# Linear attention ahead of an MLP: queries laid out by feature block and transposed on VectorE, key sums and token sums in column halves of the array

## The reference

```python
# 1: linear attention, per batch and head
q_s = exp(q - max(q, over the 64 features));  q_s /= sum(q_s, over the features) + 1e-9
k_s = exp(k - max(k, over the 576 tokens));   k_s /= sum(k_s, over the tokens) + 1e-9
kv  = k_s^T v                    # 64 x 64 per head
x   = q_s kv                     # 576 x 64 per head; the heads side by side give 576 x 512
# 2: x = x + relu(layernorm(x) * g @ w_ch1) @ w_ch2           (512 -> 2048 -> 512)
# 3: four experts, each a 64-wide causal attention over x; the best two of four by a gate are added
```

## Time and profile before

| | |
|---|---|
| median of three runs | 1400.9 us |
| the profiled execution | 1399.72 us, its span 1397.9 us |
| mean granted TensorE clock | 0.984 |
| PE busy | 1328.8 us, 95% |
| VectorE (DVE) busy | 663.0 us, 47% |
| ScalarE (ACT) busy | 498.0 us, 36% |
| GpSimd (POOL) busy | 229.6 us, 16% |
| DMA | 70.48 MB, 147018 packets, 126704 of them under 512 B |

### The profile page before, as it was taken

The page is one execution under the profiler, slowest core; times in us unless marked ns, Lnnn a source line. Parts: engine busy times, 40 slices in busy tenths (PEclk is TensorE's granted clock), DMA queues, the critical chain, the costliest instruction groups (busy, mean ns, idle before and its releaser), DMA issues.

```text
span 1397.9 us, 19591 instructions
## 1 busy us (share of the span) xinstructions
PE 1328.8 (95%) x7392; PEld 1153.6 (83%) x7392; DVE 663.0 (47%) x1628; ACT 498.0 (36%) x1092; POOL 229.6 (16%) x260
## 2 busy tenths in 40 slices
PE   4699999999999999999999999998799999999996
PEld 3577888888888888888888888887789999999984
DVE  5776344244234244244244122113677767767662
ACT  3343122122122122122122111112456666666663
POOL 0221000000000000000000000012555535543231
PEclk9899999999999999999999999999899999999998
DMA  8441410410500500600600100302112012101101
GB/s 158 125 103 67 94 35 0 105 33 8 113 17 0 128 10 8 128 1 0 136 1 8 61 0 9 97 1 77 41 35 69 24 46 69 42 28 35 34 31 38
DMA packets 147018, 70.48 MB, mean 50 GB/s; under 512 B 126704, under 2 KB 130800, under 8 KB 146928
## 3 DMA queue, kind: packets, MB, share of 16 engines
q1 hardware_dynamic: 140672, 67.66, 19.5%
q10 hardware_dynamic: 6256, 1.57, 0.7%
HBM read 49.29 MB, written 19.92 MB: 50 GB/s over the span
## 4 chain that ended last, share of the span: by engine, by line
PE 89%; DVE 4%; issue 3%; ACT 1%; POOL 1%; SPq 1%; DMA 1%; POOLq 0%; DVEq 0%; ACTq 0%
PE hb L1207 28%; PE yb L1306 27%; PE sc L1207 19%; PE ob L1444 3%; PE tb L1426 3%; PE pa L1207 2%; PE pa L1242 2%; PE yb L1294 1%; PE pa L1270 1%; PE pa L1256 1%; DVE w_lo L889 1%; DMA qsb<-in_q_dram 1%; POOL prob L635 1%; PE yb L1336 0%; SPq L415 0%
## 5 line engine op out<-in xcount | busy, mean ns | idle before, releaser
L1008 DVE SCALAR_TENSOR_TENSOR hid_lo<-hb,hid_hi 128x512 fp32r<-128x512 f32 x144 | 99.5, 691 | 454.8 <-ACT hid_hi L712 454.5
L712 ACT ACTIVATE hid_hi<-hb 128x512 fp32r<-128x512 f32 x144 | 86.0, 597 | 541.0 <-PE hb L1207 541.0
L1306 PE MATMUL yb<-hid_hi,w_hi 128*128 128x512 f32 x576 | 232.6, 404 | 0.0
L1207 PE MATMUL hb<-xn_hi,w_hi 128*128 128x512 f32 x576 | 228.2, 396 | 1.4 <-issue 1.4
L1306 PE MATMUL yb<-hid_hi,w_lo 128*128 128x512 f32 x576 | 225.0, 391 | 0.0
L1207 PE MATMUL hb<-xn_hi,w_lo 128*128 128x512 f32 x576 | 224.7, 390 | 0.0
L1306 PE MATMUL yb<-hid_lo,w_hi 128*128 128x512 f32 x576 | 224.5, 390 | 0.0
L1207 PE MATMUL hb<-xn_lo,w_hi 128*128 128x512 f32 x576 | 224.4, 390 | 0.0
L1306 PEld LDWEIGHTS yb<-hid_hi,w_lo 128*128 128x128 f32 x576 | 108.1, 188 | 23.4
L1207 PEld LDWEIGHTS hb<-xn_hi,w_lo 128*128 128x128 f32 x576 | 108.2, 188 | 23.2
L1207 PEld LDWEIGHTS hb<-xn_hi,w_hi 128*128 128x128 f32 x576 | 108.3, 188 | 23.0 <-issue 1.7
(11 more groups left out here) (180 smaller groups left out, 2366.1 us busy)
## 6 DMA issues: line engine op xcount, KB each, us to landing
y_scratch<-ysb SPq DMA_DIRECT2D x36, 256.0 KB, 2.8
qsb<-in_q_dram SPq DMA_DIRECT2D x32, 256.0 KB, 4.9
stage<-in_moe_w_ch_dram SPq DMA_DIRECT2D x16, 512.0 KB, 4.4
out_dram<-osb SPq DMA_DIRECT2D x32, 256.0 KB, 2.0
y_in<-y_scratch SPq DMA_DIRECT2D x28, 288.0 KB, 3.9
ksb<-in_k_dram SPq DMA_DIRECT2D x31, 256.0 KB, 4.5
vsb<-in_v_dram SPq DMA_DIRECT2D x28, 256.0 KB, 4.5
vsb<-in_v_dram ACTq DMA_DIRECT2D x4, 256.0 KB, 7.4
```

Of the source, the lines that this page charges most:

```text
L712: act.activation(HID[f % 2][0][:], hb[f % 2][:], ACT.Relu).then_inc(sems["hhi_a"], 1)
L1008: dve.scalar_tensor_tensor(out=lo[:], in0=hb[f % 2][:], scalar=0.0, in1=plain(hi[:]), op0=ALU.max, op1=ALU.subtract).then_inc(sems["hlo_v" ...
L1207: ins = pe.matmul(dst, l, r, start=(n == 0), stop=(n == len(terms) - 1))
L1306: ins = pe.matmul(yb[j][:], l, r, start=False, stop=(f == FT - 1 and m == 2), skip_group_check=True)
```

## The change

* **Queries.** They are loaded as `qx[128, 4, 18, 32]`: partition = (half of the heads, half of the features, token mod 32), then head in its half, block of 32 tokens, feature in its half. A DMA moves runs of 32 floats (128 B) in place of 64 (256 B), 4 DMAs of 32 partitions per batch, and each batch carries its own 576 tokens. The maximum over a row is one `tensor_reduce` over 32 features, an exchange of partition blocks (4 copies of 72 columns) and a `max`. VectorE transposes 32 x 32 blocks in place (`qT`), after which features are on partitions. TensorE's query transposes, ScalarE's copies to `qeT` and the step `qsum` are gone.
* **Key sums.** Head x * 4 + g goes to column half x of the array: 40 matmuls of 64 weight columns and 65 moving ones in place of 20 of 128 and 130. The last tile uses 64 rows.
* **Token sums.** Weights are 64 query tokens of one pair of heads (g and g + 4), the moving side `KV[:, g]` with 130 columns: kv of both heads and a column of ones for each, which yields the query sums. Per token tile 4 x 2 matmuls in alternating column halves; for the tail tile 4, all in the upper half.
* **Tokens.** A tile's step `tokens` on VectorE is an add, a reciprocal and two multiplications, and then the statistics as before. The tail goes to rows 64 to 127 of `ksb` and is stored per batch. There is no X5; `qT` stands at half 15 and `kvn` at 16 (it was 15); `ln`, `xn` and T0 to T3 stand one half earlier.
* **Buffers.** x has a buffer of its own (`xsb`), kmx lies in it; `kvbd` is one buffer `KV`; a pad keeps the place of the weights.

```diff
-        q_v = q.rearrange("(p x) h s d -> x p s h d", x=2)
+        q_v = q.rearrange("(p x) (y g) (n r) (z c) -> x p y z r g n c", x=2, y=2, r=32, z=2)
...
-        ORDER = ["kmx0", "kmx1", "kmaxT", "kbc", "ksub0", "ksub1", "qmax", "qsub0", "qsub1", "kv", "kvn", "qsum",
-                 "X0", "X1", "X2", "X3", "X4", "X5", "ln", "xn", "T0", "T1", "T2", "T3"]
+        ORDER = ["kmx0", "kmx1", "kmaxT", "kbc", "ksub0", "ksub1", "qmax", "qsub0", "qsub1", "kv", "qT", "kvn",
+                 "X0", "X1", "X2", "X3", "X4", "ln", "xn", "T0", "T1", "T2", "T3"]
...
+                for b in range(4):
+                    sp_.dma_start(qx[b * 32 : (b + 1) * 32], q_v[st[1], st[0], b // 2, b % 2]).then_inc(q_in, 16)
...
+            def store_tail(st):
+                need(sp_, "x_v", st, NT)
+                sp_.dma_start(xt_dram[st[0], st[1] * TAIL : (st[1] + 1) * TAIL], ksb[P - TAIL : P, CT, :]).then_inc(xt_out, 16)
...
+            def tokens(st, t, sums):
+                r = slice(P - ROWS[t], P)
+                need(dve, "x_mm", st, t + 1)
+                heads = sums[r, :, 0 : 4 * (HD + 1)].rearrange("p b (n c) -> p b n c", c=HD + 1)
...
+                dve.tensor_scalar(xrs[r].rearrange("p b (n o) -> p b n o", o=1), heads[:, :, :, HD : HD + 1], EPS_SUM, None, ALU.add).then_inc(sems["xrs_v"], 1)
+                need(dve, "xrs_v", st, 2 * t + 1)
+                dve.reciprocal(xrs[r], xrs[r]).then_inc(sems["xrs_v"], 1)
+                need(dve, "xrs_v", st, 2 * t + 2)
...
+                for x in range(2):
+                    ins = dve.tensor_tensor(to.rearrange("p (x b n d) -> p x b n d", x=2, b=2, n=2)[:, x], heads[:, :, x::2, 0:HD],
+                                            xrs[r, :, x::2].rearrange("p b (n o) -> p b n o", o=1).to_broadcast([ROWS[t], 2, 2, HD]), ALU.mult)
+                ins.then_inc(sems["x_v"], 1)
...
                 if s == "qmax":
+                    dve.wait_ge(q_in, st[0] * (8 * 16) + (st[1] * 64 + 64))
+                    for n in range(2):
+                        dve.tensor_reduce(qmx[:, 2 * n * NG : (2 * n + 2) * NG], qx[:, 2 * n : 2 * n + 2].rearrange("p g n c -> p (g n) c"), AX.X, ALU.max).then_inc(sems["qmx_v"], 1)
...
+                    for b in range(4):
+                        dve.tensor_copy(other[32 * b : 32 * b + 32], qmx[32 * (b ^ 1) : 32 * (b ^ 1) + 32]).then_inc(sems["qmx_v"], 1)
+                    need(dve, "qmx_v", st, 6)
+                    dve.tensor_tensor(qmx[:], qmx[:], other, ALU.max).then_inc(sems["qmx_v"], 1)
...
+                if s == "qT":
+                    for g in range(HP):
+                        need(dve, "qexp_a", st, g + 1)
+                        dve.transpose(q_part(g), q_part(g)).then_inc(sems["qT_v"], 1)
...
+            def key_sums(dst, vs, t):
+                for g in range(HP):
+                    for x in range(2):
+                        h = x * HP + g
+                        ins = pe.matmul(dst[x * HD : (x + 1) * HD, g * (HD + 1) : (g + 1) * (HD + 1)],
+                                        ksb[0 : ROWS[t], t, h * HD : (h + 1) * HD], vs[0 : ROWS[t], t, h, :],
+                                        start=(t == 0 and g == 0), stop=(t == NT - 1), skip_group_check=True)
+                return ins
...
+            def token_sums(dst, t):
+                for g in range(HP):
+                    for n in (0, 1) if t < CT else (1,):
+                        at = 4 * t + 2 * n if t < CT else 4 * t
+                        ins = pe.matmul(dst[n * HD : (n + 1) * HD, X_BANK[g], g % 2 * 2 * (HD + 1) : (g % 2 + 1) * 2 * (HD + 1)],
+                                        qx[:, g, at : at + 2, :], KV[:, g], start=True, stop=True)
+                return ins
...
                 if s[0] == "X":
...
                     t = int(s[1])
+                    need(pe, "qT_v", st, HP)
+                    if t == 0:
+                        need(pe, "kv_v", st, 2)
+                    else:
+                        need(pe, "x_v", st, t)
+                    token_sums(PA, t).then_inc(sems["x_mm"], 1)
...
             low_piece(0)
             inverse_deviation(START)
             step("xn", START)
+            tokens(START, CT, FIRST_X[CT])
```

More of the change, by code:

```diff
@@ L84, in program @@
         ksb = sb("ksb", [P, NT, D], F32, st1)
[L85 to L88, removed]
+        NG = S // 32
+        qx = sb("qx", [P, HP, NG, 32], F32, st1)
+        with ExitStack() as st:
+            kmx = sb("kmx", [P, D], F32, st)
+        xsb = sb("xsb", [P, CT, D], F32, st1)
+        KV = sb("kv", [P, HP, 2, HD + 1], F32, st1)
+        sb("pad", [P, 248], F32, st1)
         v_and_xn(0)
@@ L386, in items @@
                 return [s for s in LAST_ORDER if LAST_HALF[s] == h]
-            return [s for s in ORDER if HALF[s] == h and (s != "X5" or st[1])]
+            return [s for s in ORDER if HALF[s] == h]
         def is_last(st):
@@ L897, in token_stats, with normalize_kv @@
                 dve.bn_aggr(mv[:, t, :], bst[:, t, :]).then_inc(sems["mv_v"], 1)
-            def normalize_kv(st, first, rest):
+            def normalize_kv(st, sums):
                 need(dve, "kv_mm", st, 1)
[L901 to L904, removed]
+                kv = sums[:, 0:KVW].rearrange("p (g c) -> p g c", g=HP)
+                dve.tensor_scalar(krs[:].rearrange("p (g o) -> p g o", o=1), kv[:, :, HD : HD + 1], EPS_SUM, None, ALU.add).then_inc(sems["krs_v"], 1)
+                need(dve, "krs_v", st, 1)
+                dve.reciprocal(krs[:], krs[:]).then_inc(sems["krs_v"], 1)
@@ L905, in normalize_kv @@
                 need(dve, "krs_v", st, 2)
[L906 to L912, removed]
+                for x in range(2):
+                    h = slice(x * HD, (x + 1) * HD)
+                    dve.tensor_tensor(KV[h, :, x, 0:HD], kv[h, :, 0:HD], krs[h].rearrange("p (g o) -> p g o", o=1).to_broadcast([HD, HP, HD]), ALU.mult).then_inc(sems["kv_v"], 1)
@@ L967, in step @@
                 if s == "kvn":
-                    normalize_kv(st, pa[0][:, 0 : 3 * KVW], pa[1][:, 0:KVW])
-                if s == "qsum":
-                    need(dve, "qexp_a", st, queries(st))
-                    for t0, t1 in groups(st):
-                        dve.tensor_reduce(stat(qrs, t0, t1), per_head(qsb, t0, t1), AX.X, ALU.add).then_inc(sems["qrs_v"], 1)
-                    need(dve, "qrs_v", st, 2 + st[1])
-                    every = stat(qrs, 0, queries(st))
-                    dve.tensor_scalar(every, every, EPS_SUM, None, ALU.add).then_inc(sems["qrs_v"], 1)
-                    need(dve, "qrs_v", st, 3 + st[1])
-                    dve.reciprocal(every, every).then_inc(sems["qrs_v"], 1)
@@ L1036, in _ @@
                 step(s, START)
-            normalize_kv(START, FIRST_KV[0][:, 0 : 3 * KVW], FIRST_KV[1][:, 0:KVW])
-            step("qsum", START)
+            normalize_kv(START, FIRST_KV)
+            step("qT", START)
             for t in range(CT):
-                need(dve, "x_mm", START, t + 1)
-                need(dve, "qrs_v", START, 4)
-                dve.tensor_tensor(per_head(qsb, t, t + 1), FIRST_X[t][:].rearrange("p (h d) -> p h d", d=HD), spread(qrs, t, t + 1), ALU.mult).then_inc(sems["x_v"], 1)
-                need(dve, "x_v", START, t + 1)
-                token_stats(START, t)
+                tokens(START, t, FIRST_X[t])
             variance(START)
```

206 lines of the change are left out of this document (74 added, 132 removed).

## The result

Twenty runs of the changed kernel have a median of 1403.45 us (1400.31 to 1408.03). Nineteen of the kernel before have 1399.89 (1398.87 to 1401.77; one more run, of 2696 us, is left out). That is +3.6 us against a forecast of +0.6: inside the range of 1394 to 1412, on the slower side of the 0.2% that I called no change. The profiled execution took 1405.98 us with a span of 1403.9, so it stands 2.5 us above its median. The one before had 1399.7 and 1397.9.

A forecast was written before the change was run, and what follows sets the result against it. The prediction took the array (PE) as the bound, except where VectorE's chain leads in START and the first chunk. 1399.7 + 6.0 + 2.3 - 7.7 = 1400.3, with 1.2 for the median 1401.5 us; range 1394 to 1412.

The forecast's parts named there:

- no change: Whole kernel: a difference within about 0.2%, 2.8 us, can't be told from none; the forecast itself, chance 0.34.
- The six later chunks: Chunks after the first that carry an attention: PE time saved by cheaper key sums and token products, net -7.7 us.
- The stall of 1 us ahead of X0: Later chunks: the first token product comes 0.1 to 0.2 us late, waiting for kvn; 6 x 0.17 = 1 us.
- The start interval of 55 ns: Array passes start at most every 55 ns or so, key sums keep 4.45 us; time 1410.2 us, chance 0.20.
- The faster rival: Short passes of the key sums run at full rate, 2.3 us; time 1397.3 us, chance 0.28.
- START: Stretch before the first chunk: q's landing and VectorE's chain grow, +6.0 us (ends +3 and +10).
- The price of q: START: 14.4 ns per 128 B packet makes q's load 8.3 us instead of 4.9, +3.4 us.
- my lower end: START: q's load priced by bytes alone, +0.6 us.
- The first chunk: VectorE nearly full, token products and T0 come later, PE's saving turns into waiting; +2.3 us (ends +0.5 and +5).
- VectorE in front at double price: START and first chunk: block transposes cost twice the price, +2.4 us each; 1406.3 us, chance 0.18 shared with dear q.

The follow-up runs named there:

- warm: Changed kernel with 15 extra fp32 products of a zero matrix ahead of X0, X2 and T0 of the first chunk; 1399.46 us, 0.9989 of before.
- first_later: Changed kernel with kvn and all steps that follow it one to three halves later in the first chunk alone; 1391.56 us, 0.9942 of before.
- keysums: Kernel before with the key sums alone in column halves, keys, queries and tokens as they were; 1385.11 us, 0.9898 of before.
- best_a: keysums_all with 30 extra matmuls ahead of START's transposes; 1385.24 us, 0.9887 of before.
- ksub_first: Changed kernel with the key subtraction ahead of the query maximum in START; 1400.81 us, 1.0007 of before.
- q_256: Changed kernel with q loaded in runs of 256 B, leaving out the right placement of q; 1402.13 us, 1.0022 of before.
- keysums_all: keysums with the key subtraction first in START and a later order in the first chunk; 1381.36 us, 0.9872 of before.

## Why the prediction came out as it did

**The six later chunks, -7.7 for -8.6: right, by its mechanism.** Key sums 3.0 (measured 2.86 with the switch), token tiles 1.23 (1.30), a batch 9.5 (9.4 by the same rows). The stall of 1 us ahead of X0 did not come; without it the sum is -8.7. The start interval of 55 ns was my slower rival; passes 31 and 33 ns apart, 80 in a row, rule it out. The Trainium skill (TensorE: Matmul & The Clock Gate, Wait — 56ns, not 53.3ns?) gives some 62 ns per MATMUL where hardware decoding is off; at 31 ns per pass that bound doesn't act here. The faster rival's 2.3 for the key sums was too low, though nearer than mine on the passes alone (2.63).

**START, +6.0 for a measured +5.8: right sum by luck, wrong terms.** The profiled executions part as follows. q landed 0.8 later (predicted 3.4). qmax until ksub took 1.4 more (1.1). From there to the first token tile it was 0.5 less (1.2 less). The missing 0.7 is mostly the key sums: they ended 6.3 us after ksub began, where I had 5.65, and VectorE waited 0.6 for them. It isn't the clock of the token product, 2.01 us at a granted clock of 0.50, which was in my sum. The key sums themselves took 4.82 us at a granted clock of 1.00, while ScalarE, which feeds them, was busy for 4.96 of the 5 us from 25 to 30. The four token tiles took 2.4 more (2.0), and the fifth, behind xn, 0.1 (0.7). The first 24 MLP matmuls took 7.32 instead of 5.73, +1.6, which I didn't have. The price of q was my error of method: I drew a line through packets of 256 B and 1.7 KB and read 128 B from it. By bytes alone, my lower end, it was +0.6. Whether the 0.8 is bytes or the four DMAs of 32 partitions, of which the last is under way only from 14.51 us on (10.49 before), no run separates. The rule of the Trainium skill on reads from a 256-byte boundary (DMA: Bandwidth & Descriptors, How a descriptor splits into AXI transactions) would have given +4.8; the trace does not bear that out.

**The first chunk, +2.3 for +9.2: the step that failed.** START's 5.8 us are taken off the times here. Up to X0 it was exact: 108.1 predicted, 113.81 less START's 5.8 = 108.0 measured. From there the lag grew behind each wait. X2 came at 121.5 on that scale, not 119.4, and T0 at 144.5, not 140.2. I had priced the waits themselves and let PE go on at full speed afterwards. The rows show 6.5 us of groups at a low clock, and warm removed 6.4 of the 6.9 us by which I missed. The numbers were within reach: my own term for START says "at perhaps half clock after its pause", and I didn't carry it into a chunk for which I had forecast three pauses. The chain of this very chunk before the change had 8 passes in 2.05 us that take 0.89 elsewhere.

**VectorE in front at double price: wrong cause, right place.** Block transposes of 128 x 576 took 0.67 to 0.69 us (four in 2.67 to 2.77 in the chain), near the 0.65 that I took, where this rival had twice that. VectorE was what cost in the first chunk, but through its full order and the clock behind it.

**The total.** Profile against profile I missed by 5.4 us, 6.9 from the first chunk less 0.9 and 0.4 for the other stretches, 0.2 for START. By medians it is 1403.45 against 1401.5, 2.0 too low, and +3.6 against +0.6 as a difference, 3.0 too low. Runs of the changed kernel scatter over 7.7 us, those of before over 2.9, and the profiled one was a long one. That the total stayed inside the range by so much is luck in part, with one stretch missed by 6.9. That a fall of the clock comes or stays away in identical code (7.32 us for START's first 24 matmuls in the changed kernel, 5.72 in first_later) fits this; what decides it in a run is open. Also open are the 1.5 us that keysums gains behind the last chunk, where nothing was edited, and which of best_a's losses belong to its extra matmuls. The first chunk's code and its waits (4.1, 3.3 and 3.9 us) are the same in ksub_first and q_256, and it took 118.0 and 119.2 us there instead of 121.3. Behind the wait of 3.3 us the group took 2.95 and 2.96 us there, not 4.54, and behind that of 3.9 it took 4.34 in both, not 4.96. So 2 to 3 us of the +9.2 come and go between executions.

What the prediction never asked was what each part is worth alone. The key sums were worth 15 us, and the rest of the change, in the order it had, cost 18.

## What to carry to other kernels

Where half of a product's outputs are thrown away, as in these key sums, two products of half the width, side by side in halves of the columns, paid (4.47 to 2.48 us and 0.23 for the switch); with long passes it only broke even on the array here (a token tile 1.30 against 0.89 and 0.44 of transposes) and brought work to VectorE. A step moved behind a full engine costs its wait and the clock behind it: in the profiled execution waits of 3.3 to 4.1 us on PE cost 5.0 to 6.5 with the slow groups behind them. That is the upper end, for a wait of 3.3 us and one of 2.7 cost more than themselves in some executions and not in others. Give the one crowded chunk its own order. Time each part of a change alone, for parts of opposite sign sum to "no change".

## What the hardware showed

Products with 65 moving columns in half the array followed at 31 ns each (keysums), a full fp32 pass being 111 to 112 ns: with half of the columns in each and two side by side, 4 times the rate was the most to be had, and 3.6 were measured. Matmuls whose moving data are zeros kept the granted clock at 1.00 through waits of 3 to 4 us (warm, 0.67 without them). In best_a, with extra matmuls ahead of START's transposes, the clock was 1.00 from 46 to 54 us (0.79 in keysums_all) and fell at two later waits. Runs of 128 B moved at 209 GB/s, as 256-B runs did (209 and 215). The MLP group behind passes in halves of the columns took 0.23 to 0.27 us more than the plain 2.72, behind full passes 0.03 to 0.05 more. VectorE's transpose of 32 x 32 blocks in 128 x 576 took 0.67 to 0.69 us.
